# Attention over channels with two MLPs on one core: the first segment in whole transfers, two k squares summed on GpSimd, a regrouped fold, and v and output in one transfer each

## What is computed

```python
qn = q / (norm(q, axis=N) + 1e-6); kn = k / (norm(k, axis=N) + 1e-6)
a = softmax(kn.T @ qn / tau)            # 256 x 256
x = v @ a                               # 6016 x 256
x = (silu(x @ w_gate) * (x @ w_val)) @ w_out          # width 1536
h = x @ w_in2                                         # width 2048
out = (h * clip(h + 3, 0, 6) / 6) @ w_out2
```

## Time and profile before

| | us |
|---|---|
| median of 3 runs | 1164.02 (1162.25 to 1164.1) |
| the profiled execution | 1161.04 |
| its span | 1159.2 |
| TensorE (PE) busy | 1150.6 (99%) |
| VectorE busy | 708.4 (61%) |
| ACT busy | 269.4 (23%) |
| GpSimd busy | 76.4 (7%) |

### The profile page before, as it was taken

How to read it: one execution, slowest core, us unless ns; L and a number is a source line. 1 busy time by engine, 2 the same in 40 slices (tenths; PEclk the granted TensorE clock), 3 DMA queues, 4 the chain that set the end, 5 groups by cost and what they waited for, 6 DMA issues and landing times.

```text
span 1159.2 us, 14619 instructions
## 1 busy us (share of the span) xinstructions
PE 1150.6 (99%) x5216; PEld 967.2 (83%) x5216; DVE 708.4 (61%) x1163; ACT 269.4 (23%) x447; POOL 76.4 (7%) x48
## 2 busy tenths in 40 slices
PE   9999999999999999999999999999999999999998
PEld 8888888888888888888888888888888888888998
DVE  6786854764665575475485476466457557548555
ACT  7731211211221221221121121122122122112121
POOL 5793000000000000000000000000000000000000
PEclk9999999999999999999999999999999999999999
DMA  9642020020001002002002002001100200100100
GB/s 359 231 128 54 1 36 0 0 36 0 0 13 24 0 1 36 0 0 36 0 0 36 0 0 36 0 0 18 18 0 0 36 0 0 32 0 0 19 1 14
DMA packets 108752, 33.77 MB, mean 29 GB/s; under 512 B 98752, under 2 KB 103104, under 8 KB 108736
## 3 DMA queue, kind: packets, MB, share of 16 engines
q1 hardware_dynamic: 106416, 32.58, 11.2%
q10 hardware_dynamic: 2320, 0.98, 0.3%
HBM read 27.39 MB, written 6.16 MB: 29 GB/s over the span
## 4 chain that ended last, share of the span: by engine, by line
PE 96%; ACT 1%; DVE 1%; DMA 1%; issue 0%; ACTq 0%
PE psum L722 33%; PE psum L745 33%; PE psum L733 22%; PE psum L757 6%; PE psum L705 1%; ACT psum L372 1%; DMA tau_sb<-in_tau 1%; PE psum L625 1%; DVE sq_sum L462 1%; DMA qk_first<-in_k 0%; ACT parts_early L368 0%; ACT parts_late L368 0%; DVE psum L472 0%; PE psum L671 0%; DVE sq_sum L482 0%
## 5 line engine op out<-in xcount | busy, mean ns | idle before, releaser
L745 PE MATMUL psum<-prod,down_w 128*128 128x512 f32 (+1 forms) x1728 | 426.9, 384 | 0.0
L745 PEld LDWEIGHTS psum<-prod,down_w 128*128 128x128 f32 x1728 | 322.6, 188 | 61.7
L733 PE MATMUL psum<-yT,up_w 128*128 128x512 f32 (+1 forms) x1152 | 281.4, 385 | 0.0
L733 PEld LDWEIGHTS psum<-yT,up_w 128*128 128x128 f32 x1152 | 215.0, 188 | 41.3
L581 DVE TENSOR_TENSOR act_out<-psum,act_out 128x512 f32<-128x512 f32 (+1 forms) x144 | 97.8, 679 | 237.3 <-PE psum L722 237.2
L722 PE MATMUL psum<-vT,gate_w 128*128 128x512 f32 (+1 forms) x864 | 215.4, 384 | 0.0
L722 PE MATMUL psum<-vT,val_w 128*128 128x512 f32 (+1 forms) x864 | 215.4, 384 | 0.0
L426 ACT ACTIVATE act_out<-psum 128x512 f32<-128x512 f32 (+1 forms) x144 | 85.1, 591 | 470.5 <-PE psum L722 470.5
L722 PEld LDWEIGHTS psum<-vT,gate_w 128*128 128x128 f32 x864 | 161.3, 188 | 30.9
L722 PEld LDWEIGHTS psum<-vT,val_w 128*128 128x128 f32 x864 | 161.3, 188 | 30.9
L594 DVE SCALAR_TENSOR_TENSOR act_out<-act_out,psum 128x512 f32<-128x512 f32 (+1 forms) x192 | 129.0, 672 | 76.8 <-ACT act_out L434 76.8
(11 more groups left out here) (84 smaller groups left out, 327.3 us busy)
## 6 DMA issues: line engine op xcount, KB each, us to landing
v_in<-in_v SPq DMA_DIRECT2D x44, 128.0 KB, 3.4
out<-out_sb SPq DMA_DIRECT2D x44, 128.0 KB, 2.5
qk<-in_q SPq DMA_DIRECT2D x7, 512.0 KB, 9.4
qk<-in_k SPq DMA_DIRECT2D x7, 512.0 KB, 10.7
w_stage<-in_moe_w_out SPq DMA_DIRECT2D x7, 512.0 KB, 3.9
w_stage<-in_moe_w_in SPq DMA_DIRECT2D x4, 512.0 KB, 3.6
qk_more<-in_q SPq DMA_DIRECT2D x3, 512.0 KB, 10.7
qk_more<-in_k SPq DMA_DIRECT2D x3, 512.0 KB, 12.0
```

What stands on the lines that cost most here:

```text
L733: end = mm(HID[j % 4][:, 0:n], up2_w[:, part, b, j * P:(j + 1) * P], yT[:, m, b, 0:n], start=(part, m, b) == (0, 0, 0), stop=(part, m, b) ...
L745: end = mm(banks[h][:, 0:n], w[:, part, j, h * P:(h + 1) * P], prod[:, c % 4, m, 0:n], start=j == 0 and (part, m) == PASSES[0], stop=False)
```

## The change

- **First chunks and segment 0.** One transfer of 256 KB for q and one for k, then one of 512 KB each. TensorE waits for the whole of each.
- **k squares of segments 8 and 9** (`POOL_SUMS`). ACT writes them to SBUF, into the two still unused staging places `w_stage`. GpSimd adds them and folds the sum to 256 columns in two steps. VectorE has 18 adds of segments in place of 20 (`ADDS`). The norm products of k take this sum as a second operand: six products in place of four. SP issues the first piece into `w_stage` only after the norm products.
- **Fold.** The groups run half 0 and half 1 over blocks 0 to 3, then half 0 and half 1 over blocks 4 and 5. `turn_exp(1)` stands ahead of group 3 (`TURNED_AT`). The first tile waits for 6, 8 and 12 low parts in place of 8, 10 and 12.
- **v and output.** One transfer for each load and store in place of four.

```diff
+    POOL_SUMS = range(8, 10)
-        first_loaded = [sem(f"first_loaded{c}") for c in range(FIRST)]
+        first_loaded = sem("first_loaded")
-        rest_loaded = sem("rest_loaded")
+        k_folded = sem("k_folded")
-        GROUPS_OF_FOLD = [(h, i) for h in range(KC) for i in range(len(UP_BLOCKS))]
+        GROUPS_OF_FOLD = [(h, i) for blocks in (range(4), range(4, 6)) for h in range(KC) for i in blocks]
+        TURNED_AT = 3
+        ADDS = [(s, h) for s in range(FULL_SEGS - 1) for h in range(2) if h == 0 or s not in POOL_SUMS]
+
+        def adds_before(s, h):
+            return max((i + 1 for i, (at, x) in enumerate(ADDS) if x == h and at < s), default=0)
+
+        def folded_squares(s):
+            return w_stage[:, POOL_SUMS.index(s), :]
...
-            for g in range(GROUPS):
-                queue.dma_start(out_last[0][g][:, h::KC, :], out_sb[g * SQUARE:(g + 1) * SQUARE, h:LAST // SQUARE * KC:KC, :]
-                                ).then_inc(out_stored, 16)
+            queue.dma_start(out_last[0][:, :, h::KC, :], out_sb[:, h:LAST // SQUARE * KC:KC, :]
+                            ).then_inc(out_stored, 16)
...
-            for c in range(FIRST):
-                sp.dma_start(qk_first[:, 0, c * C:(c + 1) * C], q_seg[:, c * C:(c + 1) * C]).then_inc(first_loaded[c], 16)
-            load(sp, 0, 0, 0, WIDE * C, seg_loaded[0])
-            load(sp, 0, 0, WIDE * C, SEG * C, rest_loaded)
+            sp.dma_start(qk_first[:, 0, :], q_seg[:, 0:FIRST * C]).then_inc(first_loaded, 16)
+            load(sp, 0, 0)
...
             def load_v(rows, tokens):
-                for g in range(GROUPS):
-                    sp.dma_start(v_in[g * SQUARE:(g + 1) * SQUARE, 0:tokens // SQUARE * KC, :],
-                                 rows[g]).then_inc(v_loaded, 16)
+                sp.dma_start(v_in[:, 0:tokens // SQUARE * KC, :], rows).then_inc(v_loaded, 16)
...
             load_v(v_full[0], BANK)
+            sp.wait_ge(norms_summed, 1)
...
-                for g in range(GROUPS):
-                    sp.dma_start(rows[g], out_sb[g * SQUARE:(g + 1) * SQUARE, 0:tokens // SQUARE * KC, :]
-                                 ).then_inc(out_stored, 16)
+                sp.dma_start(rows, out_sb[:, 0:tokens // SQUARE * KC, :]).then_inc(out_stored, 16)
...
+            pool.wait_ge(squared, 2 * POOL_SUMS.stop)
+            nc.gpsimd.tensor_tensor(folded_squares(8), folded_squares(8), folded_squares(9), ALU.add).then_inc(k_folded, 1)
+            for i, width in enumerate((2 * C, C)):
+                pool.wait_ge(k_folded, i + 1)
+                nc.gpsimd.tensor_tensor(folded_squares(8)[:, 0:width], folded_squares(8)[:, 0:width],
+                                        folded_squares(8)[:, width:2 * width], ALU.add).then_inc(k_folded, 1)
...
                 for h in range(2):
+                    kept = SQ[h] if h == 0 or s not in POOL_SUMS else folded_squares(s)
                     if s >= 1:
-                        act.wait_ge(squares_added, 2 * (s - 1) + h + 1)
-                    nc.scalar.activation(SQ[h], slot(s)[:, h, :], ACT.Square).then_inc(squared, 1)
+                        act.wait_ge(squares_added, adds_before(s, h))
+                    nc.scalar.activation(kept, slot(s)[:, h, :], ACT.Square).then_inc(squared, 1)
...
-            pe.wait_ge(squares_added, 2 * (FULL_SEGS - 1) + 8)
+            pe.wait_ge(squares_added, len(ADDS) + 8)
+            pe.wait_ge(k_folded, 3)
             for x in range(2 * KC):
-                end = mm(NORMS[:, x:x + 1], sq_sum[:, x // KC, x % KC * P:(x % KC + 1) * P], ones[:, 0:1],
-                         start=True, stop=True)
+                cols = slice(x % KC * P, (x % KC + 1) * P)
+                sums = (sq_sum[:, 0, cols],) if x < KC else (sq_sum[:, 1, cols], folded_squares(8)[:, cols])
+                for i, squares_of in enumerate(sums):
+                    end = mm(NORMS[:, x:x + 1], squares_of, ones[:, 0:1], start=i == 0, stop=i == len(sums) - 1)
...
-                    pe.wait_ge(fold_ready, len(UP_BLOCKS) + 2 + 2 * (j // 4))
+                    pe.wait_ge(fold_ready, (6, 8, 12)[j // 4])
```

More of the change, by code:

```diff
@@ L231, in up_split_cols, with load @@
             return first_up[:, g, part, :, n * BANK:(n + 1) * BANK]
+        ADDS = [(s, h) for s in range(FULL_SEGS - 1) for h in range(2) if h == 0 or s not in POOL_SUMS]
[3 more added lines that the diff above has]
+            return w_stage[:, POOL_SUMS.index(s), :]
         TURNS = (4, 6)
         TURNED = (2, 4)
-        def load(queue, s, x, begin, end, loaded):
-            at = seg_at(s)
-            queue.dma_start(slot(s)[:, x, begin:end], (q_seg, k_seg)[x][:, at + begin:at + end]).then_inc(loaded, 16)
+        def load(queue, s, x):
+            width = seg_chunks(s) * C
+            queue.dma_start(slot(s)[:, x, 0:width], (q_seg, k_seg)[x][:, seg_at(s):seg_at(s) + width]
+                            ).then_inc(seg_loaded[s], 16)
         def slot(s):
@@ L343, in _ @@
         def _(act):
-            for c in range(FIRST):
-                act.dma_start(qk_first[:, 1, c * C:(c + 1) * C], k_seg[:, c * C:(c + 1) * C]).then_inc(first_loaded[c], 16)
-            load(act, 0, 1, 0, WIDE * C, seg_loaded[0])
-            load(act, 0, 1, WIDE * C, SEG * C, rest_loaded)
+            act.dma_start(qk_first[:, 1, :], k_seg[:, 0:FIRST * C]).then_inc(first_loaded, 16)
+            load(act, 0, 1)
             def table_of(function):
@@ L353, in _ @@
             table_of(ACT.Sqrt)
-            for c in range(FIRST):
-                act.wait_ge(first_loaded[c], 32)
+            act.wait_ge(first_loaded, 32)
             for h in range(2):
@@ L455, in _ @@
             dve.wait_ge(sums_cleared, 1)
-            for s in range(FULL_SEGS - 1):
-                for h in range(2):
-                    dve.wait_ge(squared, 2 * s + h + 1)
-                    if s >= 1:
-                        dve.wait_ge(squares_added, 2 * (s - 1) + h + 1)
-                    nc.vector.tensor_tensor(sq_sum[:, h, :], SQ[h], sq_sum[:, h, :], ALU.add).then_inc(squares_added, 1)
-            added = 2 * (FULL_SEGS - 1)
+            for s, h in ADDS:
+                dve.wait_ge(squared, 2 * s + h + 1)
+                if s >= 1:
+                    dve.wait_ge(squares_added, adds_before(s, h))
+                nc.vector.tensor_tensor(sq_sum[:, h, :], SQ[h], sq_sum[:, h, :], ALU.add).then_inc(squares_added, 1)
+            added = len(ADDS)
             half = 2 * C
@@ L650, in _ @@
             stay_awake(AWAKE_START)
+            pe.wait_ge(first_loaded, 32)
             for c in range(FIRST):
-                pe.wait_ge(first_loaded[c], 32)
                 for h in range(KC):
                     product(h, qk_first[:, 0, c * C:(c + 1) * C], qk_first[:, 1, c * C:(c + 1) * C], start=c == 0)
-            wide(0, range(WIDE), range(KC))
-            pe.wait_ge(rest_loaded, 32)
-            wide(0, range(WIDE, SEG), range(KC)).then_inc(seg_multiplied, 1)
+            wide(0, range(SEG), range(KC)).then_inc(seg_multiplied, 1)
             for s in SPLIT:
```

20 lines of the change are left out of this document (9 added, 11 removed).

## The result

The changed kernel takes 1169.48 us (median of 6 runs, 1168.31 to 1172.21), the kernel before 1162.79 us (6 runs, 1160.88 to 1164.1). The ratio is 1.0062, with a 95% interval of 1.0045 to 1.0079: slower by 0.6%, clear of noise (the medians lie 6.7 us apart). The profiled execution took 1171.9 us on a span of 1170.1, 10.9 us over the span of before.

What follows compares the result with a forecast made beforehand. TensorE was taken as the bound (96% of the chain), so only its idle stretches and the tail count. Terms -1.0 + 0 + 0.5 + 0.3 + 1.8 + 5.6 = +7.2 us on the 1164.02 median gave 1171.2, range 1162.5 to 1176.

Steps and rivals of the forecast that it cites:

- four engines in the tail: Last stores: an outermost count of 4 leaves four of 16 DMA engines carrying a single transfer; chance 0.73.
- first segment whole: Head: larger first pieces bring segment 0 earlier and speed the norm chain; -1.0 us, bounds +0.3 to -1.8.
- k sums on GpSimd: Head: VectorE loses two adds, but the q squares' chain still sets the last add; zero gain, at most 0.1 us.
- norm products: Head, on TensorE's path: two more products in four rows; +0.5 us, bounds 0.3 and 0.5.
- fold order: Fold: the first group of half 1 comes fifth and waits for its expT; +0.3 us, bounds 0 and 0.5.
- v lands late: Head: first v on four engines lands near 53.1, delaying VectorE and TensorE's fifth fold group; +1.8 us, bounds 0 to +4.8.
- tail: After the last products: 393 KB of output on four engines ends the span later; +5.6 us, bounds +3.9 to +8.6.
- Rival A: Single DMAs for v and output keep all 16 engines; 1163.0 us, no measurable change; chance 0.21.
- rival B: Tail and starting stream: pieces cost more than bytes, so both get faster; sum -3.0, 1161.0 us; chance 0.06.
- the stretch ahead of the norms: Head: TensorE's idle time before the norm products stays around 1 us although VectorE has two adds less.

Runs made afterwards that it cites:

- tau later: Against four transfers again: VectorE waits for tau only behind the adds of segment 9, tau loaded as before; 1163.27 us, ratio to the kernel before 1.0006.
- tau first: Against four transfers again: tau's DMA is ACT's first, ahead of k's first chunks; 1162.75 us, ratio to the kernel before 1.0004.
- four transfers again: Against the changed kernel: v and the output move by one DMA for each group again; 1163.13 us, ratio to the kernel before 1.0006.
- only the tail in four: Against the changed kernel: only the two last half stores in four transfers each, v and tile stores single; 1163.29 us, ratio to the kernel before 1.0016.
- kernel without the sums: Against four transfers again: VectorE adds all twenty squares again, with four norm sums of one part each; 1162.91 us, ratio to the kernel before 1.0008.
- two-transfer kernel: Against the changed kernel: each last half stored by two transfers of two groups, outermost count 2; 1176.66 us in a single run.

## Why the prediction was right

The forecast was 1171.2 within 1162.5 to 1176, with 0.73 on slower; the median is 1169.5. The mechanism that carried it, four engines in the tail, is the one that was found. The sum fits better than its terms, though. Part of the 1.7 us between forecast and median is the base: +7.2 was put on 1164.02, the median of three runs, and the median of six is 1162.79.

| term | forecast, us | measured, us | where |
|---|---|---|---|
| first segment whole | -1.0 (+0.3 to -1.8) | 0.0 | last add ends 41.35, before 41.37 |
| k sums on GpSimd | 0 | about 0 | 1.0006 with, 1.0008 without |
| norm products | +0.5 | +0.45 | 1.36 for 0.91 at full clock |
| fold order | +0.3 (0 to 0.5) | +0.36 | 17.16 for 16.80 |
| v lands late | +1.8 (0 to 4.8) | 0 | fold 17.16 with one DMA and with four, at full clock |
| tail | +5.6 (3.9 to 8.6) | +6.8 | 12.0 for 5.2 |
| clock behind the norms | not in it | 0 to +3.3 | by execution |

**Tail: right, and sized too low by 1.2.** SP's first packets flow 1.2 us after the issue (1157.78, 1159.0), where I had estimated 1.25. They flow for 9.9 us, where the sum used 9.3 (9.9 GB/s for each engine), and behind the last packet another 1.2 us pass, not 0.6: each of the two makes 0.6 of the miss. The windows' share, which I expected near 0.25, is 0.19 to 0.41, and 0.41 also where one queue flows alone; at full flow it goes over 1. So it doesn't count engines. The rate is the better witness: 43 to 48 GB/s at a count of 4, 22 at a count of 2. Rival A (16 engines, 1163.0) and rival B (faster) are out: neither the tail's flow nor that of a full tile (150 to 200 us) exceeds 54 GB/s for v or output.

**v: the step that failed is the rate.** I took 11.2 GB/s for each engine, from rows where 16 engines store and load at once and are fed by four transfers. Alone on four engines, the load flows at 54, 13.5 each, which was my bound at 13. With it, VectorE has v at 51.78, where I had forecast 53.1. It does wait 0.23 for it in the profile with the full clock. By my reckoning (4.5 us from the turns to expT's low part, wanted at 55.8) that is still some 0.5 too late for TensorE, and the fold shows none of that. In the changed kernel's own profile VectorE turns v at 54.95 without waiting, since the clock had moved everything back by 3.3 us: one loss was the cover of another.

**Head: the step that failed is that the norm chain moves with the stream.** The stream did speed up (417 GB/s where it was 217), ACT's first full square is at 7.42, and TensorE was earlier for a while. Two things ate it. tau did not come near 10; it stayed at 11.66, and its own pieces slow the stream in which it is, so that of 0.6 MB of head start at 8 us only 0.1 MB is left at 12. And behind it waits a second limit, which I didn't look for: segment 6. ACT's cast of it stands at 24.99 in the kernel before with no idle time ahead, which looks like an engine that is busy, and where a run waits for its data, these are there 0.2 us earlier (24.77 in the second profile of this head, 24.80 in *tau later*). I had bounded the gain by the slack at segment 2 (0.56) and not at every later segment. Taking VectorE's wait for tau away (*tau later*, *tau first*) moved the last add by 0.1 us at most.

**Sums and norm rows: right.** The waits of 1.15 between VectorE's adds are the hand-over that had been worked out (2.38 us a segment for the q square alone), and GpSimd's sum is ready at 39.2, forecast 39.0, two us ahead of VectorE.

**Fold order: right,** 0.36 for 0.3. Where it arises is not shown in full: the chain has a gap of 0.07 us before the seventh row behind the two transposes, where the fifth group starts with expT of half 1.

**Not foreseen: the clock.** I named the stretch ahead of the norms and expected it to stay at around 1 us. It was 1.52, and I priced what it does to the clock at nothing. In half of the executions that cost 1.7 to 3.5 us more. Whether the change makes the stretch longer is open, as the unchanged head has shown 0.99 and 1.58. But the fall comes more often with the changed head: the mean clock is 0.998 or less in 29 of 43 runs of *four transfers again*, *only the tail in four*, *tau later* and the kernel without the sums together, and in 27 of 87 runs of the kernel before, beside all the experiments. The forecast of the median was near with luck: -1.0 and +1.8 both were 0, the tail and the clock were larger, and the base was 1.2 too high. What carries over is the tail.

## What to carry to other kernels

When DMAs are merged, look at the outermost count of both sides in the order of the instructions: merging four transfers of 32 partitions into one whose outermost count is 4 leaves four of sixteen engines at work, which costs nothing in the middle of a run and everything behind the last product. An earlier start of a chain is worth no more than the smallest slack it has to any later arrival, so go through all of them, the ones without idle time too. And a stretch in which TensorE stands still may cost more than its length: in some executions the clock falls behind it, here for up to 3.3 us in all.

## What the runs showed of the hardware

- **The rate goes by the outermost count.** 4: 43 to 48 GB/s for stores and 54 for loads, by 128-byte pieces; 2: 22 GB/s for stores, also with two transfers on each of two queues.
- **The second queue's packets come late.** In the tail SP's store moved 33 to 36 GB/s alone for 3 us from 1159. ACT's, issued at 1158.75, had its first packets only just before 1162. And the issue of a transfer that stands behind a long one holds its engine: SP's issues of v, most behind a full tile's store, took 11.6 us (median of 12), ACT's two stores in the tail of the two-transfer kernel 8.98 together.
- **A tiny transfer slows a large stream.** One value spread to 128 partitions takes 7 us among full-size pieces (issue 4.59, landed by 11.66) and drops 420 GB/s to 226 for 2 us and 328 for 2 more. First in the queue it drops the first 4 us instead, and is there by 4.84.
- **Code loading is a transfer too.** In the changed kernel between 20 and 26 us one 16 KB packet of instructions takes 1.0% of 16 engines' time:

```profile
q1 hardware_dynamic: 683, 2.49, 101.7%
q8 instruction: 1, 0.02, 1.0%
```

  1.0% of 16 x 6 us is 0.96 us on one engine. Every kernel here has such a packet between 20.5 and 24.5 us. That it holds segment 6 up by the one engine is not shown: it stands between 20.5 and 21 in *tau later* and between 22.5 and 23 in *tau first*, and segment 6 is there at 24.80 and at 24.86.
- **The clock falls in some executions and not in others, on the same idle time.** Two profiles with TensorE idle for 1.54 and 1.61 us ahead of the norms: tiles at 68.10 with a half-clock stretch of 3.4 us in the one, 66.38 at full clock in the other; the kernel before's head, idle for 1.58, is at full clock too (65.59). Six of 27 runs of the kernel before beside the last experiments lie at 1163.1 to 1164.0, with 0.997 or 0.998. At 0.21 us of idle time none of 11 was under 0.999. Where it fell, the stretch at half clock was 3.4 us (*four transfers again*, no sums) or 6.8 us (the changed kernel, *tau later*), and cost half of that. Windows of TensorE in the two kernels, first four transfers again, then only the tail in four:

```profile
44.00:46.00 2.00, 2.00 (x6) 1.63 (x5) 0.00 (x0) 1.99 (x4) 2.00 (x1) 0.50 0.66 104
```

```profile
44.00:46.00 2.00, 2.00 (x13) 1.82 (x12) 0.84 (x2) 1.99 (x4) 2.00 (x2) 1.00 0.38 62
```
